# Gates ahead of vals, one group for each of the last three tiles, and ScalarE's exponents as a step of their own

## The reference, cut to what matters

```python
# 1: attention at full length with a band mask, plus attention on 4-fold pooled q, k, v -> x (2304 x 512)
# 2: gated layer
gate = 1.0 / (1.0 + np.exp(-(x @ w_gate)))         # 512 -> 1536
val = x @ w_val
y = gate * val @ w_out                             # 1536 -> 512
# 3: soft mixture of 8 experts with 4 slots each
logits = y @ phi                                   # 2304 x 32
d = softmax(logits, over the tokens)
slot_input = d.T @ y                               # 32 x 512
slot_out[e] = maximum(slot_input[e] @ w1[e], 0) @ w2[e]
c = softmax(logits, over the slots)
out = c @ slot_out                                 # 2304 x 512
```

## Time and profile before

| | |
|---|---|
| median of three runs | 551.37 us (551.12 to 553.83) |
| the profiled execution | 553.79 us, its span 552.0 us |
| busy TensorE, VectorE, ScalarE, GpSimd | 96%, 41%, 35%, 19% |
| TensorE granted clock, mean | 0.985 |
| DMA | 71.00 MB, mean 129 GB/s |
| DMA in slices 33 to 40 (13.8 us each) | 262 275 215 397 394 400 192 342 GB/s |
| chain of waits, by engine | PE 85%, DMA 6%, SPq 2%, DVE 2% |

### The profile page before, as it was taken

One profiled execution on the slowest core, in us unless ns is written; L12 is line 12 of the kernel. 1 busy time (PEld: TensorE's weight loads), 2 busy tenths in 40 slices (PEclk: granted clock), 3 DMA queues, 4 the chain that ended last, 5 costly groups with the idle time before them and its releaser, 6 DMA issues.

```text
span 552.0 us, 11786 instructions
## 1 busy us (share of the span) xinstructions
PE 528.6 (96%) x4770; PEld 404.1 (73%) x4770; DVE 225.4 (41%) x484; ACT 195.8 (35%) x530; POOL 106.8 (19%) x171
## 2 busy tenths in 40 slices
PE   5989999999999999999999999999999999999982
PEld 4768778877887787878777877878777788854431
DVE  0977965343643446253353527432223110140113
ACT  3757754242443243424233425233122212231022
POOL 8556253221212123112121212100000000000000
PEclk9979999999999999999999999999999999999997
DMA  9966963210311122011111110107006077599959
GB/s 207 231 159 153 341 131 89 67 44 14 77 47 45 45 45 67 23 47 44 47 44 45 45 47 0 27 1 287 18 0 213 17 262 275 215 397 394 400 192 342
DMA packets 86709, 71.00 MB, mean 129 GB/s; under 512 B 61312, under 2 KB 65920, under 8 KB 86656
## 3 DMA queue, kind: packets, MB, share of 16 engines
q1 hardware_dynamic: 86656, 70.25, 41.5%
HBM read 65.52 MB, written 4.72 MB: 127 GB/s over the span
## 4 chain that ended last, share of the span: by engine, by line
PE 85%; DMA 6%; SPq 2%; DVE 2%; issue 1%; ACT 1%; POOL 1%; DVEq 0%; ACTq 0%; POOLq 0%
PE gateb L1036 26%; PE valb L1036 26%; PE unitb L1046 4%; DMA ew_low<-in_moe_w_dram 3%; PE unitb L944 3%; PE unitb L989 3%; PE unitb L937 3%; PE unitb L1060 2%; PE unitb L1085 2%; DMA v<-in_v_dram 2%; PE unitb L973 2%; PE unitb L952 1%; PE unitb L1136 1%; PE unitb L979 1%; PE gateb L1154 1%
## 5 line engine op out<-in xcount | busy, mean ns | idle before, releaser
L1036 PE MATMUL valb<-w_hl,xhl 128*128 128x512 f32 x648 | 162.1, 399 | 0.0
L1036 PE MATMUL gateb<-w_hl,xhl 128*128 128x512 f32 x648 | 161.7, 398 | 0.0
L1036 PEld LDWEIGHTS gateb<-w_hl,xhl 128*128 128x128 f32 x648 | 118.3, 188 | 28.9 <-issue 4.1
L1036 PEld LDWEIGHTS valb<-w_hl,xhl 128*128 128x128 f32 x648 | 118.4, 188 | 25.0 <-issue 1.4
L851 DVE SCALAR_TENSOR_TENSOR hid<-hid,valb 128x512 f32<-128x512 f32 x54 | 37.1, 687 | 121.8 <-PE valb L1036 121.7
L730 ACT ACTIVATE hid<-gateb 128x512 f32<-128x512 f32 x54 | 32.2, 597 | 143.6 <-PE gateb L1036 143.6
L647 POOL TENSOR_TENSOR vd<-v 72x256 f32<-72x256 f32 x16 | 13.6, 850 | 103.6 <-PE unitb L973 87.5
L843 DVE TENSOR_TENSOR xhl<-xraw,xhl 128x512 fp32r<-128x512 f32 x18 | 12.8, 709 | 48.9 <-ACT xhl L658 48.8
L1046 PE MATMUL unitb<-ident,hid 128*128 128x128 f32 x216 | 31.9, 272 | 0.0
L658 ACT ACTIVATE hT<-unitb 128x512 f32<-128x512 f32 x54 | 31.7, 592 | 0.3 <-PE unitb L1046 0.3
L1046 PEld LDWEIGHTS unitb<-ident,hid 128*128 128x128 f32 x216 | 26.5, 140 | 6.8 <-issue 0.4
(11 more groups left out here) (179 smaller groups left out, 659.3 us busy)
## 6 DMA issues: line engine op xcount, KB each, us to landing
ew_low<-in_moe_w_dram SPq DMA_DIRECT2D x19, 1024.0 KB, 12.1
ew_high<-in_moe_w_dram SPq DMA_DIRECT2D x13, 1024.0 KB, 8.2
qtok<-in_q_dram SPq DMA_DIRECT2D x32, 144.0 KB, 2.7
ktok<-in_k_dram SPq DMA_DIRECT2D x32, 144.0 KB, 2.9
v<-in_v_dram SPq DMA_DIRECT2D x32, 144.0 KB
out_dram<-outs SPq DMA_DIRECT2D x18, 256.0 KB, 3.0
vloc<-in_v_dram SPq DMA_DIRECT2D x32, 112.0 KB
xraw<-in_moe_w_out_dram SPq DMA_DIRECT2D x12, 256.0 KB, 4.7
```

Of the source, the lines that this page charges most:

```text
L1036: last = mm(bank[:, :], xhl[:, i % NX, x, kk, :], w_hl[:, c, m, w, kk, :], start=j == 0, stop=j == len(order) - 1)
```

## The change

The chunks 1 and 2 of the last three tiles are worked on as all six gates, then all six vals. Tile 16 and tile 17 are groups of their own; `hT` places are given by `hT_place`. ScalarE's exponents are a step LX, placed apart from LS in the tail, and `alpha` has two places. The last val is cut after 4 and after 9 of its 12 products for TR (16,2) with LS 8, and for LG 9. The order in which the weights' places are filled follows. The eight clock-keeping products behind the last LS are gone, and SL of the second last group has four behind it like the last. The list from gate (15,1) on is now:

```diff
@@ -84,9 +84,8 @@
     t0 = tiles - 3
     ff = [(name, (i, c)) for i in range(t0) for c in range(chunks) for name in ("gate", "val")]
     ff += [(name, (i, 0)) for i in range(t0, tiles) for name in ("gate", "val")]
-    for c in range(1, chunks):
-        ff += [("gate", (t0, c)), ("val", (t0, c)), ("gate", (t0 + 1, c)), ("gate", (t0 + 2, c)), ("val", (t0 + 1, c)),
-               ("val", (t0 + 2, c))]
+
+    ff += [(name, (i, c)) for name in ("gate", "val") for c in range(1, chunks) for i in range(t0, tiles)]
     place_of = {s: n for n, s in enumerate(ff)}
 
 
@@ -109,22 +108,23 @@
     for g, (first, size) in enumerate(groups):
         n = place_of[("val", (first + size - 1, chunks - 1))]
         if first + size < t0:
-            for at, name in ((2, "LG"), (3, "LS"), (5, "ELT"), (6, "SL")):
-                put(n + at, (name, g))
-
-    last_c, g = chunks - 1, len(groups) - 3
+            for at, *names in ((2, "LG"), (3, "LS", "LX"), (5, "ELT"), (6, "SL")):
+                put(n + at, *[(name, g) for name in names])
+
+
+    last_c, g = chunks - 1, len(groups) - 4
     n = place_of[("gate", (t0, 0))]
-    for at, *those in ((1, ("LG", g)), (2, ("LS", g)), (3, ("ELT", g), ("TR", (t0, 0)), ("SL", g)), (6, ("TR", (t0 + 2, 0)))):
+    for at, *those in ((1, ("LG", g)), (2, ("LS", g), ("LX", g)), (3, ("ELT", g), ("TR", (t0, 0)), ("SL", g)), (6, ("TR", (t0 + 1, 0)))):
         put(n + at, *those)
     for c in range(1, last_c):
-        n = place_of[("gate", (t0, c))]
-        put(n + 2, ("TR", (t0, c)))
-        put(n + 6, ("TR", (t0 + 2, c)))
-    n = place_of[("gate", (t0, last_c))]
-    for at, *those in ((2, ("TR", (t0, last_c))), (3, ("LG", g + 1)), (4, ("LS", g + 1), *[("TR", (t0 + 1, c)) for c in range(chunks)]),
-                       (5, ("ELT", g + 1), ("LG0", g + 2), ("TR", (t0 + 2, last_c)), ("SL", g + 1)),
-                       (6, ("LG", g + 2)), (7, ("LS", g + 2)), (8, ("ELT", g + 2)), (9, ("SL", g + 2))):
-        put(n + at, *those)
+        put(place_of[("val", (t0, c))] + 1, ("TR", (t0, c)))
+        put(place_of[("val", (t0 + 1, c))] + 1, ("TR", (t0 + 1, c)))
+    n = place_of[("val", (t0, last_c))]
+    put(n - 1, ("LG0", g + 1))
+    put(n, *[("TR", (t0 + 2, c)) for c in range(last_c)], ("TR", (t0, last_c)))
+    put(n + 1, ("LG", g + 1), ("TR", (t0 + 1, last_c)), ("LS", g + 1), ("LX", g + 1), ("LG", g + 2))
+    put(n + 2, ("LS", g + 2), ("ELT", g + 1), ("LG0", g + 3), ("TR", (t0 + 2, last_c)), ("SL", g + 1), ("LX", g + 2), ("LG", g + 3),
+        ("ELT", g + 2), ("LS", g + 3), ("SL", g + 2), ("LX", g + 3), ("ELT", g + 3), ("SL", g + 3))
 
 
 
@@ -172,6 +172,13 @@
     k = body.index(("gate", (1, 0)))
     assert set(body[:k]) <= set(head) | set(tile_0)
     return head, tile_0 + body[k:]
+
+
+def inside_items(tiles, chunks, groups_n):
+
+    c, g = chunks - 1, groups_n - 3
+    last = ("val", (tiles - 1, c))
+    return {(last, 4): (("TR", (tiles - 2, c)), ("LS", g)), (last, 9): (("LG", g + 1),)}
 
 
 def place(head, body, narrow):
@@ -250,7 +257,7 @@
     CG = 4
     SW = FF // CG
     GT = 2
-    GROUPS = [(i, GT) for i in range(0, TILES - 4, GT)] + [(TILES - 4, 1), (TILES - 3, 1), (TILES - 2, GT)]
+    GROUPS = [(i, GT) for i in range(0, TILES - 4, GT)] + [(i, 1) for i in range(TILES - 4, TILES)]
     GROUPS_T = len(GROUPS)
     group_of = {first + t: (g, t) for g, (first, size) in enumerate(GROUPS) for t in range(size)}
     RING = 2 * S
@@ -270,10 +277,16 @@
     ff_n = {arg: n for n, arg in enumerate(arg for name, arg in body if name == "gate")}
     assert [arg for name, arg in body if name == "val"] == list(ff_n)
 
+    inside = inside_items(TILES, FC, GROUPS_T)
+
+    def hT_place(i):
+
+        return 1 if i == TILES - 2 else group_of[i][1]
+
     def hT_before(i):
 
-        g, t = group_of[i]
-        return max((n for n in range(g) if GROUPS[n][1] > t), default=None)
+        return max((group_of[n][0] for n in range(i) if group_of[n][0] < group_of[i][0] and hT_place(n) == hT_place(i)),
+                   default=None)
 
     ctx = ExitStack()
     with ctx:
@@ -294,7 +307,7 @@
         part_max = sb("part_max", [P, 1])
         neg_max = sb("neg_max", [P, 2])
         max_step = sb("max_step", [P, 1])
-        alpha = sb("alpha", [P, 1])
+        alpha = sb("alpha", [P, 2])
         part_sum = sb("part_sum", [P, 1])
         c_max = sb("c_max", [P, GT])
         c_sum = sb("c_sum", [P, GT])
@@ -392,7 +405,8 @@
         W_PLACE = (ATT_BYTES + X_BYTES + SPARE) // (4 * HALF_TILE)
         X_PLACE = W_PLACE + W_PLACES
         VAL_LOW, VAL_HIGH = X_PLACE - 1, X_PLACE - 2
-        first_places = [*range(WO_SLOTS, VAL_HIGH), X_PLACE + 1, VAL_LOW, VAL_HIGH, X_PLACE, *range(X_PLACE + 2, SLOTS)]
+        first_places = [*range(WO_SLOTS, W_PLACE + 6), VAL_HIGH - 2, VAL_HIGH - 1, W_PLACE + 6, W_PLACE + 7,
+                        X_PLACE + 1, VAL_LOW, VAL_HIGH, X_PLACE, *range(X_PLACE + 2, SLOTS)]
 
         def place_of_tile(i):
             if i < FIRST:
@@ -414,6 +428,7 @@
         const_done = sem("const_done")
         rep_done = sem("rep_done")
         mask_step = sem("mask_step")
+        lg_begun = sem("lg_begun")
         zero_done = sem("zero_done")
         phi_in = sem("phi_in")
         w_in = [sem(f"w_in{i}") for i in range(len(w_pieces))]
@@ -732,8 +747,10 @@
             elif name == "TR":
                 i, c = arg
                 wait_unit(act, s)
-                t = group_of[i][1]
-                if c == 0 and hT_before(i) is not None:
+                t = hT_place(i)
+                if i == TILES - 1 and c < FC - 1:
+                    act.wait_ge(lg_begun, 1)
+                elif c == (FC - 1 if i == TILES - 1 else 0) and hT_before(i) is not None:
                     wait_unit(act, ("LG", hT_before(i)))
                 copy(hT[:, 4 * c:4 * c + 4, t * P:(t + 1) * P], ub[:, :].rearrange("p (f n) -> p f n", f=4)).then_inc(free, 1)
             elif name == "LG":
@@ -742,14 +759,16 @@
                     wait_unit(act, ("LS", arg - 1))
                 tok = GROUPS[arg][1] * P
                 copy(l4[:, 0:tok], ub[:, 0:tok]).then_inc(free, 1)
-            elif name == "LS":
+            elif name == "LX":
+                ub, free = banks[at["LS", arg][1]], bank_free[at["LS", arg][1]]
                 act.wait_ge(lmax_step, 3 * arg + 3)
                 if arg > 0:
                     wait_unit(act, ("ELT", arg - 1))
                     act.wait_ge(slot_sum, arg)
-                    wait_free(act, ("SL", arg - 1))
+                if arg > 1:
+                    wait_free(act, ("SL", arg - 2))
                 tok = GROUPS[arg][1] * P
-                nc.scalar.activation(alpha[:], max_step[:], ACT.Exp).then_inc(alpha_done, 1)
+                nc.scalar.activation(alpha[:, arg % 2:arg % 2 + 1], max_step[:], ACT.Exp).then_inc(alpha_done, 1)
                 nc.scalar.activation(el[:, 0:tok], ub[:, 0:tok], ACT.Exp, bias=neg_max[:, arg % 2:arg % 2 + 1],
                                      accum_out=part_sum[:]).then_inc(el_done, 1)
 
@@ -866,7 +885,7 @@
                 logits = ub[:, 0:size * P].rearrange("p (t n) -> p t n", t=size)[:, :, NS:2 * NS]
                 wait_free(dve, ("LS", arg))
                 dve.wait_ge(alpha_done, arg + 1)
-                nc.vector.scalar_tensor_tensor(out=run_sum[:], in0=run_sum[:], scalar=alpha[:], in1=part_sum[:],
+                nc.vector.scalar_tensor_tensor(out=run_sum[:], in0=run_sum[:], scalar=alpha[:, arg % 2:arg % 2 + 1], in1=part_sum[:],
                                                op0=ALU.mult, op1=ALU.add).then_inc(slot_sum, 1)
                 dve.wait_ge(etok_done, arg + 1)
                 nc.vector.reduce_max(c_max[:, 0:size], logits, AX.X).then_inc(c_step, 1)
@@ -876,7 +895,7 @@
             elif name == "SL":
                 def add_up():
                     wait_unit(dve, s)
-                    nc.vector.scalar_tensor_tensor(out=acc[:, :], in0=acc[:, :], scalar=alpha[:], in1=ub[:, 0:SW],
+                    nc.vector.scalar_tensor_tensor(out=acc[:, :], in0=acc[:, :], scalar=alpha[:, arg % 2:arg % 2 + 1], in1=ub[:, 0:SW],
                                                    op0=ALU.mult, op1=ALU.add).then_inc(free, 1)
 
                 first, size = GROUPS[arg]
@@ -1037,6 +1056,8 @@
                               start=j == 0, stop=j == len(order) - 1)
                     if j == lows - 1:
                         last.then_inc(low_used, 1)
+                    for between in inside.get((s, j + 1), ()):
+                        pe_step(pe, between)
                 last.then_inc((gate_ready, val_ready)[m], 1)
             elif name == "TR":
                 i, c = arg
@@ -1050,15 +1071,17 @@
                 first, size = GROUPS[arg]
                 ub = banks[at["LG", arg][1]]
                 for r in range(FC):
-                    if arg == GROUPS_T - 1 and (r < FC - 1) != (name == "LG0"):
+                    if arg in (GROUPS_T - 1, GROUPS_T - 3) and (r < FC - 1) != (name == "LG0"):
```

(11 more changed lines are left out.)

## The result

The changed kernel took 552.87 us (median of 20 runs, 551.10 to 560.55), the kernel before 550.14 in the same comparison (20 runs, 548.50 to 554.17). The ratio is 1.0047, 95% interval 1.0029 to 1.0064: 2.6 us slower, 1.6 to 3.5. (Ratios leave out single runs far above the rest of their kernel, such as the 560.55.) The prediction said 552.9, with +1.5 us for the change.

A forecast was written before the change was run, and what follows sets the result against it. TensorE's relay and the weight stream were taken to bound the end within 0.3 us. Last val +1.05 and relay 10.35 against 9.6 put the transposes 1.8 later; less 0.3, +1.5 on the 551.37 median: 552.9, range 550.4 to 555.6.

The forecast's parts named there:

- The transposes of the sums 1.8 later: End of the relay on TensorE: the transposes of the sums start at 495.83 instead of 494.02, about 1.8 us later.
- Part 1: Order of the last gates and vals on TensorE: the last val, (17,2), ends 1.05 us later, at 485.48.
- Part 3: Relay from the last val to the sums' transposes: 10.35 us against 9.6, with SL 8 waiting for LX 9's bank.
- rival A's second form: Relay: if only SL 8 doesn't hold LG 10 back, 1.6 go, no change, 551.3; within a shared chance of 0.18.
- The weights off the path: End of the expert weight stream: last transfer lands at 532 to 532.6, wanted at 534.4, so its 0.3 us wait goes.
- From the sums' transposes on nothing is changed: Experts and output, behind the relay: no change from the edit, so 0.
- The removed fillers cost nothing: Clock-keeping products taken out of the relay: no cost in themselves, as what was under them was waiting; clock priced apart.
- Rival B: Relay: TensorE idles about 2.2 us, the clock drops to half, adding 1.5 to 4 us, 3 taken: 556; chance 0.14.
- One reading was off: Reading of the profile before: slices 32 to 40 alone show DMA traffic at its ceiling.

The follow-up runs named there:

- e_moved: Changed kernel with LG 9 behind the last val, SL 8 on LG 9's bank, ELT 8's exponent later, fewer fillers, 12 start products: 1.0033 of the kernel before.
- e_bank: Changed kernel with SL 8 on the second gate bank instead of the one LS 9 holds: relay 8.62 instead of 9.91 us, 1.0023 of the kernel before.
- e_pad: Changed kernel with eight one-column products added at TensorE's start: output stage 18.17 us, 1.0037 of the kernel before.
- e_oldw: Changed kernel with the weights' places filled in the old order: 1.0065 of the kernel before.
- e_k8: Changed kernel with the eight clock-keeping products back behind the last LS: relay 12.93 us, 1.0073 of the kernel before.
- e_nofill: Changed kernel without clock-keeping products from the last LG to the last SL: relay 10.19 us, 1.0046 of the kernel before.

## Why the prediction was right, and where it was not

**The transposes of the sums 1.8 later**: measured 1.50 + 0.31 = 1.81, as predicted. But two errors of 0.45 cancel in it.
- *Part 1* said +1.05 and it is +1.50. Counted in both timelines from each row's start to the next row's start, the difference is: logits +0.94 (0.79 was priced), transposes of `hid` +0.44 (0.16 was priced), gates and vals +0.18 (0.1 was priced), LS +0.09 and ELT -0.16 (neither was priced; ELT 8 moved behind the last val). The term for LG 9, 0.79, is right (479.71 to 480.50). Not priced was that LG 8 was cut too, into LG0 (0.57, 468.63 to 469.20) and LG (0.36, 476.41 to 476.77), where it had cost 0.79 in one. The largest miss is in the transposes: the three sets behind val (15,2) took 1.41 instead of 1.23, about as priced, but the sets that LG0 8 and LS 8 follow hold TensorE for 0.53 and 0.43, where a set followed by a gate or val holds it for 0.35. The three pieces of the last val take 1.03, 1.33 and 0.81 up to the next work, 3.17 in all, against 2.84 for one piece (481.43 to 484.27); with one cut less (e_moved) it is 3.03.
- *Part 3* said 10.35 and it is 9.90. The order of waits came out step by step: exponent of ELT 8, copy, LX 9, bank, SL 8, LG 10, LS 10, LX 10. SL 8 started 3.33 behind the last val's end instead of 3.63, since ScalarE's operations overlap by 0.1 each where they don't depend on one another, and SL 8 held TensorE for 0.67, not 0.80. e_bank shows that this bank alone was worth 1.29; as rival A's second form would have it, this takes the relay below the old one.

**The weights off the path**: right, 0.28 came back, as the 0.3 said. The slack was not 1.9 us. The last transfer landed at 529.67, and TensorE took it up at 529.95; in e_pad and e_oldw it waited again. The two transfers behind the wait for all banks did land late, as laid out, but the second landed 3.9 us behind the first instead of 2.6 (496.4 and 500.3), and the eleven behind it took 29.4 instead of 28.6. "The stream is off the path" held by a hair, not by the margin given.

**"From the sums' transposes on nothing is changed"** is the step that failed. The output stage grew by 0.96, from code loading: TensorE's program has 18 more matmul records (nine products) and as many weight loads, and with this length a 16 KB transfer of the instruction queue falls among the output issues. It is a part of the change's price in this form, though nothing of its idea. With it the sum is 2.48, and the timed difference 2.6; the prediction's +1.5 was short by just this, and lies under the interval of 1.6 to 3.5. That the absolute 552.9 was met within 0.1 is luck: the three runs of before at hand had a median 1.2 above that of twenty, which made up for the output stage.

**"The removed fillers cost nothing"**: their removal didn't, but for another reason than given. In the old order they filled a wait; in the new one the same eight would have stood ahead of SL 9 and cost about 1.6 at full clock, the 3.0 of e_k8 less the 1.4 of its low clock.

**Rival B** was given 0.14. Its mechanism is real, at half to three quarters of the price given (3): 1.4 us in e_k8, and 2.3 in e_nofill (10.19 against the 9.3 laid out, and 1.45 behind). In the changed kernel's two profiles it did not strike, though the stop that exposes a kernel to it is in both. That the forecast came out rather than B is so in part by chance.

**One reading was off**, with nothing resting on it: DMA traffic was said to be at its ceiling in slices 32 to 40. The table of before has 215 to 275 GB/s in slices 33 to 35 and about 400 from 36 to 38.

## What to carry to other kernels

When a list of steps is reordered by hand, count through which buffer each step gets, and look for a step whose buffer is held by something that now comes late: here that one count was worth more than all else in the relay. Cutting a run of products to slip others in costs at each cut, here 0.14 to 0.19 us. Products put in at the start of a program are not free in any number: here eight or nine cost nothing there, twelve about 1 us. And compare stages between fixed marks, not spans, where the start of the kernel wanders by more than the effect.

## What was not expected of the hardware

- The length of one engine's program moved a 16 KB transfer of the instruction queue into the output stage: the longest DMA issue took 0.93 to 1.71 us instead of 0.65, and the stage 0.7 to 1.2 us more. With 16 matmul records more than in the changed kernel, or 22 fewer, it costs 0.1 at most (18.17 and 18.07).
- The granted clock fell to 0.50 within 1.2 us of a stop of 1.83 to 1.84 us in two profiles and stayed at 1.00 after the same stop, behind the same work, in four others.
- The part ahead of the last split of x spread over 5 us (413.5 to 418.6) between profiles; low clock stretches between 34 and 53 us explain a part of it, the twelve products of e_moved another, the rest is open. It isn't the change: with the sums of the table, the two medians put this part within 0.3 us of each other (552.87 - 135.88 and 550.14 - 133.40, each with what lies around the span).
